# A two-layer kernel with a causal convolution in front: layer 1's 128-column down products in float32r parts, low parts made by transfers

## The chip, the cores and the metric
The kernel runs on one core of one Trainium2 chip. The time is that of the device in microseconds, from one launch to its end; three runs of the kernel before give a median of 1350.51 us (1350.42 to 1352.89). All operands and results are float32 in HBM.

## What is computed
The input is x (2, 4096, 192). A depthwise causal convolution with 7 taps comes first, its weights a softmax over the taps of each of 8 heads of 24 features. Two layers follow on the 8192 tokens, each 192 to 2048 to 192:

```python
x1 = conv(x, softmax(weight))
h = x1 @ w_in1;  g1 = h * (1 / (1 + exp(-1.702 * h)));  x2 = g1 @ w_out1
h = x2 @ w_in2
P = a0 + a1*h + a2*h**2 + a3*h**3
Q = 1 + abs(b0)*abs(h) + abs(b1)*h**2
out = (P / (Q + 1e-6)) @ w_out2
```

## The kernel before
Tokens are handled in 16 tiles of 512 (index i), and the 2048 hidden features in 16 blocks of 128, two at a time, a duo. A tile has eight steps (s = 0 to 7), one for each duo; n = 8 i + s numbers them. All tensors stand with features on the partitions and tokens along the row.

Step n does, on TensorE in this order (`step`, L365): the up products of layer 1 for duo n (`up`, L285: per block four full products of float32r, then `up_rest`, L294, a 64-row one), those of layer 2 for duo n - 10, and then the down products, of layer 2 for duo n - 12 and of layer 1 for duo n - 1. A down product has a 64-column part (`down_b`, L314, fp32; both layers side by side in one bank) and a 128-column part. For layer 2 the latter is fp32 (`down_a`, L299). For layer 1 it is `down_a` in two duos of eight and in all of tile 0, and `down_a_split` (L306) in the six duos of `S_SPLIT`: there the first block is one fp32 product (L309), and the second is made of three float32r products (L310 to L312), of the high and low parts of weights and g: hi x hi, lo x hi, hi x lo. An fp32 product stands in the trace as two records.

ScalarE reads h of layer 2 three times (`linear`, L510; Square, L525; Abs, L527), does layer 1's Gelu (L533), rounds the second block of g to float32r (`g_hi`, L536), and for the ratio P/Q makes two squares (L574, L576) and a seed of the reciprocal from Q's bits (L581). VectorE makes the numerator (L713, L715), Q (L716), two steps of the ratio (L735, L739, the latter writes g of layer 2), the last factor (L748), `g_lo` = g - g_hi (L764), and the taps of the next tile's convolution (`conv_ops`, L638, spread over the steps by the table `CONV_AT`). GpSimd makes m = Q x seed once a step (L858), which needs ScalarE's Abs and is needed by L574. SP's queue holds only loads and stores of tiles (`tile_io`, L257). Layer 2's input needs layer 1's sums: high parts by ScalarE (L540) and VectorE (L706), low parts by VectorE (L708, L742), at s = 0.

x is transposed on TensorE at s = 7 (half 0) and s = 0 (half 1), the result y at s = 5 and 6; ScalarE evacuates them in the same step, between its Gelu and L574, and splits x1 at s = 6. `y_a` and `y_b` are copied from the sums at s = 3. Tiles 0 to 2 and the last ones are written out; the ten tiles between run in a loop of two tiles (`Fori`) on every engine. The last ten duos of layer 2 run alone.

All orders are written out by hand through the numbers at the top (lags, `S_...`, `CONV_AT`) and semaphores; there is no scheduler.

## Time and profile before

| | before |
|---|---|
| median of 3 runs | 1350.51 us (1350.42 to 1352.89) |
| the profiled execution | 1351.36 us, its span 1348.9 us |
| instructions | 15463 |
| VectorE busy | 1180.0 us in 1323 instructions |
| ScalarE busy | 1023.6 us in 1235 instructions |
| GpSimd busy | 322.5 us in 147 instructions |
| bytes moved by DMA | 20.56 MB, mean 15 GB/s |

The span is the time from the first to the last instruction on the core; all times in rows count from its start. Busy time is the union of the instructions of an engine; matmuls overlap, so that distances between their starts say more than their lengths.

### The profile page before, as it was taken

Reading aid. Unit: us, or ns where it says so; the run is one execution under the profiler, and the core shown is the slowest. Engines: PE = TensorE matmul, PEld = TensorE weight load, DVE = VectorE, ACT = ScalarE, POOL = GpSimd, SP = SyncE. Lnnn points to the kernel's source line nnn. Section 1 sums busy time; section 2 is a strip of 40 time slices with the busy share of each in tenths; the row PEclk is TensorE's granted clock in tenths of the full one; section 3 lists DMA queues with packets and bytes.
Section 4 is the critical chain, followed back from the end, with each engine's and each line's share of the span. In section 5 each row is a group of like instructions: output and inputs, shape, how many; then the busy total and the mean of one; then the engine's idle time right before and its main releaser. Section 6 shows DMA issues by size and latency. Waiting matters only on the chain. (4 is left out here: it accounts for less than half of the span.)

```text
span 1348.9 us, 15463 instructions
## 1 busy us (share of the span) xinstructions
PE 1306.8 (97%) x4902; PEld 714.3 (53%) x4902; DVE 1180.0 (87%) x1323; ACT 1023.6 (76%) x1235; POOL 322.5 (24%) x147
## 2 busy tenths in 40 slices
PE   5998999999999999999999999999999999999896
PEld 3554555555555555555555555555555555555432
DVE  4469898989989898998989999898999989987897
ACT  4357778787877877787877878788787877877675
POOL 2312222222222222222222222222222222222231
PEclk9999999999999999999999999999999999999899
DMA  7200000000000000000000000000000000000000
GB/s 190 76 0 0 12 1 24 1 24 1 12 12 0 24 0 24 0 12 12 0 24 0 23 0 12 12 0 24 0 12 12 1 12 1 12 0 12 1 12 12
DMA packets 32922, 20.56 MB, mean 15 GB/s; under 512 B 10337, under 2 KB 30817, under 8 KB 32865
## 3 DMA queue, kind: packets, MB, share of 16 engines
q1 hardware_dynamic: 32388, 19.93, 5.3%
q8 instruction: 19, 0.31, 0.1%
q14 instruction: 38, 0.31, 0.1%
q10 hardware_dynamic: 477, 0.01, 0.0%
HBM read 13.64 MB, written 6.29 MB: 15 GB/s over the span
## 5 line engine op out<-in xcount | busy, mean ns | idle before, releaser
L858 POOL TENSOR_TENSOR work<-work 128x1024 f32<-128x1024 f32 x127 | 302.9, 2385 | 973.8 <-ACT work L527 927.1
L303 PE MATMUL acc_a<-g,down 128*128 128x512 f32 x664 | 312.3, 600 | 0.0
L317 PE MATMUL acc_b<-g,down 128*64 128x512 f32 x992 | 256.9, 608 | 17.4 <-DVE g L739 13.5
L514 ACT ACTIVATE work<-h,par 128x1024 f32<-128x1024 f32 x128 | 142.7, 1115 | 160.2 <-PE h L297 159.7
L289 PE MATMUL h<-x_a_hi,up_a_hi 128*128 128x512 f32 x512 | 234.3, 458 | 8.8 <-DVE x_a_lo L742 4.9
L713 DVE TENSOR_TENSOR work<-work,h 128x1024 f32<-128x1024 f32 x128 | 156.2, 1221 | 76.3 <-ACT work L527 75.1
L574 ACT ACTIVATE work<-work 128x1024 f32<-128x1024 f32 x127 | 134.9, 1062 | 96.3 <-POOL work L858 96.0
L290 PE MATMUL h<-x_a_lo,up_a_hi 128*128 128x512 f32 x512 | 201.0, 393 | 0.0
L291 PE MATMUL h<-x_a_hi,up_a_lo 128*128 128x512 f32 x512 | 200.9, 392 | 0.0
L292 PE MATMUL h<-x_b,up_b_hi 128*128 128x512 f32 x512 | 200.5, 392 | 0.0
L303 PEld LDWEIGHTS acc_a<-g,down 128*128 128x128 f32 x664 | 121.6, 189 | 142.8 <-issue 134.6
L715 DVE SCALAR_TENSOR_TENSOR work<-work,par,h 128x1024 f32<-128x1024 f32 x128 | 163.9, 1281 | 4.5
L739 DVE SCALAR_TENSOR_TENSOR g<-work 128x1024 f32<-128x1024 f32 x127 | 155.7, 1226 | 12.5 <-DVE work L735 1.9
L748 DVE SCALAR_TENSOR_TENSOR work<-work,par 128x1024 f32<-128x1024 f32 x128 | 163.7, 1279 | 1.1 <-ACT work L581 1.1
L735 DVE SCALAR_TENSOR_TENSOR work<-work 128x1024 f32<-128x1024 f32 x127 | 154.8, 1219 | 7.1 <-ACT work L574 7.0
L716 DVE SCALAR_TENSOR_TENSOR work<-work 128x1024 f32<-128x1024 f32 x128 | 156.1, 1220 | 0.0
L533 ACT ACTIVATE g<-h 128x1024 f32<-128x1024 f32 x128 | 132.5, 1035 | 30.2 <-PE h L297 30.2
L317 PEld LDWEIGHTS acc_b<-g,down 128*64 128x64 f32 x992 | 65.7, 136 | 143.4 <-issue 124.0
L581 ACT ACTIVATE work<-work 128x1024 int32<-128x1024 int32 x128 | 133.6, 1044 | 7.9 <-DVE work L716 7.9
L576 ACT ACTIVATE work<-work 128x1024 f32<-128x1024 f32 x127 | 132.6, 1044 | 0.0
L527 ACT ACTIVATE work<-h 128x1024 f32<-128x1024 f32 x128 | 131.1, 1024 | 0.0
L525 ACT ACTIVATE work<-h 128x1024 f32<-128x1024 f32 x128 | 129.9, 1015 | 0.0
(117 smaller groups left out, 1418.3 us busy)
## 6 DMA issues: line engine op xcount, KB each, us to landing
out<-y_out SPq DMA_DIRECT2D x15, 384.0 KB, 2.5
x_in_a<-in_x SPq DMA_DIRECT2D x16, 256.0 KB, 2.8
down<-in_moe_w_out SPq DMA_DIRECT2D x8, 384.0 KB, 6.3
...
work<-in_moe_w_in SPq DMA_DIRECT2D x8, 256.0 KB, 4.3
...
wts<-in_weight ACTq DMA_DIRECT2D x2, 0.4 KB
```

What stands on the lines that cost most here:

```text
L289: mm(h, l.up_a_hi[:, cols], l.x_a_hi[:, p, :], start=True, stop=False)
L290: mm(h, l.up_a_hi[:, cols], l.x_a_lo[:, p, :], start=False, stop=False)
L291: mm(h, l.up_a_lo[:, cols], l.x_a_hi[:, p, :], start=False, stop=False)
L292: mm(h, l.up_b_hi[:, cols], l.x_b[:, p, :], start=False, stop=False)
L303: last = mm(l.acc_a[:], l.down[:, f, 0:P], l.g[:, slot, k, :], start=f == 0, stop=f == STEPS - 1)
L317: return mm(acc_b[l.acc_row:l.acc_row + DB, :], l.down[:, f, P:D], l.g[:, slot, k, :], start=f == 0, stop=f == STEPS - 1)
L713: tt(tu, tu, h, ALU.mult).then_inc(t2_ready, 1)
L715: stt(tu, tu, par[:, 1:2], h, ALU.add, ALU.mult).then_inc(t3_ready, 1)
L716: stt(sk, ab, 1.0 + 1e-6, sk, ALU.add, ALU.add).then_inc(q_ready, 1)
L739: stt(gv, s2, d2, zv, ALU.add, ALU.mult).then_inc(g2_ready, 1)
L748: stt(zu, tu, par[:, 0:1], seed, ALU.add, ALU.mult).then_inc(z1_ready, 1)
L858: tt(m, sq[(s - LAG_RATIO) % 2], seed, ALU.mult).then_inc(m_ready, 1)
```

## The change
All 128-column down products of layer 1 are made of float32r parts, for both blocks of every duo and in tile 0 too: six products in place of four or two. The signs are turned: the weights have parts `down_nhi` = -hi, `down_nlo` and `down_hi`, and g has `g_nhi` = -hi. The low part of g is `g_low` = g + g_nhi. In tile 0 VectorE adds it; from tile 1 on two plain transfers on SP's queue copy g to `g_low`, and two adding transfers on GpSimd's queue add `g_nhi` onto it. Layer 2's fp32 products now stand ahead of layer 1's. z shares t1's buffers, and s2 those of sq, which frees room. Transpositions of x go to s = 5 and 6, of y to s = 0 and 1 of the tile after; ScalarE evacuates at the end of the step before. x1 is split at s = 4 and 5. The taps stand at s = 6 and 7 (of the tile after next) and s = 1, 2, 3. The loops are gone.

```diff
-S_XT = (7, 0)
-S_X1 = 6
+S_XT = (5, 6)
+S_X1_B = 4
+S_X1_A = 5
+S_X1_LO = 5
-S_SPLIT = (1, 2, 3, 4, 5, 7)
-S_YT = (5, 6)
+S_YT = (0, 1)
+S_LOAD = 3
-    CONV_AT = (0, 3, 8, 11, 14, 17, NX, NX, NX)
-    CONV_AT_FIRST = (0, 0, 0, 0, 7, 14, NX, NX, NX)
+    CONV_HEAD = {6: (0, 7), 7: (7, 10)}
+    CONV_AT = (10, 10, 13, 16, NX, NX, NX, NX, NX)
+    CONV_AT_FIRST = (0, 0, 0, 3, 10, NX, NX, NX, NX)
...
+            for n in range(END):
+                i, s = n // DUOS, n % DUOS
+                if live(n) and n >= DUOS:
+                    sp.wait_ge(g1_ready, n + 1)
+                    for k in range(2):
+                        sp.dma_start(g_low[:, n % 2, k, :].bitcast(F32), L1.g[:, n % 2, k, :]).then_inc(g1_copied[2 * (n % 2) + k], 16)
...
-            def down_a_split(d, slot):
-                acc = L1.acc_a[:]
-                mm(acc, L1.down[:, 2 * d, 0:P], L1.g[:, slot, 0, :], start=d == 0, stop=False)
-                mm(acc, down_hi[:, d, :], g_hi[:, slot, :], start=False, stop=False)
-                mm(acc, down_lo[:, d, :], g_hi[:, slot, :], start=False, stop=False)
-                return mm(acc, down_hi[:, d, :], g_lo[:, slot, :], start=False, stop=d == DUOS - 1)
+            def down_a_parts(v, slot):
+                acc = L1.acc_a[:]
+                for k in range(2):
+                    f = 2 * (v % DUOS) + k
+                    if v >= DUOS:
+                        pe.wait_ge(g1_low[2 * slot + k], 16 * ((v - DUOS) // 2 + 1))
+                    elif k == 0:
+                        pe.wait_ge(g1_low_first, v + 1)
+                    mm(acc, down_nhi[:, f, :], g_nhi[:, slot, k, :], start=f == 0, stop=False)
+                    mm(acc, down_nlo[:, f, :], g_nhi[:, slot, k, :], start=False, stop=False)
+                    done = mm(acc, down_hi[:, f, :], g_low[:, slot, k, :], start=False, stop=f == STEPS - 1)
+                return done
...
+            def linear(n, k):
+                act.wait_ge(h2_ready, k + 1)
+                if k - 2 + LAG_UP2 >= TOTAL - 1:
+                    wait(act, z1_ready, k - 1)
+                else:
+                    wait(act, g2_ready, k - 1)
...
+                    act.wait_ge(g1_ready, n + 1)
+                    fn(g_nhi[:, n % 2, :, :], L1.g[:, n % 2, :, :], ACT.Copy, scale=-1.0).then_inc(g1_nhi_ready, 1)
...
+                if n < DUOS:
+                    dve.wait_ge(g1_nhi_ready, n + 1)
+                    tt(g_low[:, n % 2, :, :], L1.g[:, n % 2, :, :], g_nhi[:, n % 2, :, :].bitcast(F32), ALU.add)\
+                        .then_inc(g1_low_first, 1)
+                    if s < CHUNKS:
+                        down_lo(s)
...
+                if live(n) and n >= DUOS:
+                    pool.wait_ge(g1_nhi_ready, n + 1)
+                    for k in range(2):
+                        pool.wait_ge(g1_copied[2 * (n % 2) + k], 16 * ((n - DUOS) // 2 + 1))
+                        pool.dma_start(g_low[:, n % 2, k, :], g_nhi[:, n % 2, k, :], accum_op=ALU.add)\
+                            .then_inc(g1_low[2 * (n % 2) + k], 16)
```

TensorE's down products of one middle step, with numbers for the layer or the bank behind a name (acc_a1 is layer 1's sum). Before, a split step:

```order
L317 MATMUL acc_b<-g2,down2 64x512 [waits g2_ready,g1_ready]
L317 MATMUL acc_b<-g1,down1 64x512
L317 MATMUL acc_b<-g2,down2 64x512
L317 MATMUL acc_b<-g1,down1 64x512
L309 MATMUL acc_a1<-g1,down1 128x512 [waits g1_lo_ready]
L310 MATMUL acc_a1<-g_hi,down_hi 128x512
L311 MATMUL acc_a1<-g_hi,down_lo 128x512
L312 MATMUL acc_a1<-g_lo,down_hi 128x512
L303 MATMUL acc_a2<-g2,down2 128x512 x2
```

Of the change, the same place:

```order
L350 MATMUL acc_b<-g2,down2 64x512 [waits g2_ready,g1_ready]
L350 MATMUL acc_b<-g1,down_b1 64x512
L350 MATMUL acc_b<-g2,down2 64x512
L350 MATMUL acc_b<-g1,down_b1 64x512
L330 MATMUL acc_a2<-g2,down2 128x512 x2
L343 MATMUL acc_a1<-g_nhi,down_nhi 128x512 [waits g1_low_0]
L344 MATMUL acc_a1<-g_nhi,down_nlo 128x512
L345 MATMUL acc_a1<-g_low,down_hi 128x512
L343 MATMUL acc_a1<-g_nhi,down_nhi 128x512 [waits g1_low_1]
L344 MATMUL acc_a1<-g_nhi,down_nlo 128x512
L345 MATMUL acc_a1<-g_low,down_hi 128x512
```

Layer 2's pair moved ahead of layer 1's products, which wait once for each half's transfer.

GpSimd's queue in the change, two middle steps (work<-work is m; before, only those rows stood here):

```order
L885 TENSOR_TENSOR work<-work 128x1024 [waits s2_ready,h2_read,seed_ready]
L891 DMA g_low<-g_nhi 128x512 [waits g1_copied_0,g1_nhi_ready]
L891 DMA g_low<-g_nhi 128x512 [waits g1_copied_1]
L885 TENSOR_TENSOR work<-work 128x1024 [waits s2_ready,h2_read,seed_ready]
L891 DMA g_low<-g_nhi 128x512 [waits g1_copied_2,g1_nhi_ready]
L891 DMA g_low<-g_nhi 128x512 [waits g1_copied_3]
```

Each m now stands behind the two adding transfers of the step before, and they behind SP's copies.

## Rows read from the trace of the kernel before
**Rows 1.** The page, busy time and share of the span of each engine.
```profile
PE 1306.8 (97%) x4902; PEld 714.3 (53%) x4902; DVE 1180.0 (87%) x1323; ACT 1023.6 (76%) x1235; POOL 322.5 (24%) x147
PEclk9999999999999999999999999999999999999899
```
**Rows 2.** Windows (stretch: length, busy PE, PEld, DVE, ACT, POOL, clock, DMA): middle tile, tile 2, tile 1.
```profile
617.06:696.51 79.45, 79.14 (x309) 44.12 (x308) 72.64 (x82) 63.28 (x76) 19.02 (x8) 1.00 0.03 10
140.61:219.94 79.33, 79.09 (x307) 44.17 (x307) 71.93 (x82) 63.23 (x76) 19.00 (x8) 1.00 0.04 11
64.57:140.61 76.04, 70.49 (x257) 38.38 (x257) 62.03 (x68) 48.16 (x55) 13.02 (x5) 1.00 0.03 9
```
**Rows 3.** Timeline of TensorE, two middle steps: start, length, line [idle before <- releaser].
```profile
640.98 1.88 PE L303 MATMUL acc_a<-g,down 128*128 128x512 f32 x4
642.92 0.39 PE L290 MATMUL h<-x_a_lo,up_a_hi 128*128 128x512 f32 x1
...
646.45 0.73 PE L297 MATMUL h<-x_b,up_b_lo 64*128 64x512 f32 x4
647.11 1.94 PE L317 MATMUL acc_b<-g,down 128*64 128x512 f32 x8
...
656.11 0.73 PE L297 MATMUL h<-x_b,up_b_lo 64*128 64x512 f32 x4
```
**Rows 4.** Timeline of ScalarE and VectorE in one step (s = 2 of a middle tile).
```profile
637.59 1.11 ACT L514 ACTIVATE work<-h,par 128x1024 f32<-128x1024 f32 x1 [1.69 <-PE h L297]
...
640.41 1.04 ACT L533 ACTIVATE g<-h 128x1024 f32<-128x1024 f32 x1
640.63 1.22 DVE L713 TENSOR_TENSOR work<-work,h 128x1024 f32<-128x1024 f32 x1 [0.59 <-ACT work L527]
641.47 0.63 ACT L536 ACTIVATE g_hi<-g 128x512 fp32r<-128x512 f32 x1
643.01 1.07 ACT L574 ACTIVATE work<-work 128x1024 f32<-128x1024 f32 x1 [0.90 <-POOL work L858]
645.53 1.23 DVE L739 SCALAR_TENSOR_TENSOR g<-work 128x1024 f32<-128x1024 f32 x1
646.67 1.28 DVE L748 SCALAR_TENSOR_TENSOR work<-work,par 128x1024 f32<-128x1024 f32 x1
```
**Rows 5.** Timeline at s = 0, the step after it, and s = 4.
```profile
617.95 1.12 ACT L514 ACTIVATE work<-h,par 128x1024 f32<-128x1024 f32 x1 [1.75 <-PE h L297]
621.25 1.22 DVE L713 TENSOR_TENSOR work<-work,h 128x1024 f32<-128x1024 f32 x1
627.62 1.94 PE L317 MATMUL acc_b<-g,down 128*64 128x512 f32 x8 [0.17 <-DVE g L739]
...
656.98 0.20 PEld L317 LDWEIGHTS acc_b<-g,down 128*64 128x64 f32 x4 [0.57 <-ACT y_a L593]
```
**Rows 6.** Groups by line (busy us, mean ns | idle before).
```profile
L764 DVE TENSOR_TENSOR g_lo<-g,g_hi 128x512 fp32r<-128x512 f32 x90 | 61.6, 684 | 2.2 <-ACT g_hi L536 2.2
L841 POOL TENSOR_TENSOR up_a_lo<-work,up_a_hi 128x512 fp32r<-128x512 f32 x7 | 9.4, 1336 | 32.3 <-DVE x_b L687 17.8 <-ACT up_b_hi L508 14.5
```
**Rows 7.** DMA issues (KB each, median us to landing), and the window of the fastest transfers.
```profile
x_in_a<-in_x SPq DMA_DIRECT2D x16, 256.0 KB, 2.8
down<-in_moe_w_out SPq DMA_DIRECT2D x8, 384.0 KB, 6.3
32.00:40.00 8.00, 8.00 (x29) 3.69 (x25) 0.96 (x5) 4.76 (x8) 2.56 (x2) 1.00 0.96 282
```
**Rows 8.** Timeline of VectorE in tile 1: taps, and the numerator's first operation of two steps.
```profile
98.47 0.74 DVE L656 SCALAR_TENSOR_TENSOR conv_a<-xt_a,wts,conv_a 128x512 f32<-128x512 f32 x1
99.13 0.47 DVE L656 SCALAR_TENSOR_TENSOR conv_b<-xt_b,wts,conv_b 128x256 f32<-128x256 f32 x1
99.53 2.86 DVE L656 SCALAR_TENSOR_TENSOR conv_a<-xt_a,wts,conv_a 128x512 f32<-128x512 f32 x1
...
102.31 1.21 DVE L713 TENSOR_TENSOR work<-work,h 128x1024 f32<-128x1024 f32 x1
...
113.72 1.21 DVE L713 TENSOR_TENSOR work<-work,h 128x1024 f32<-128x1024 f32 x1
```

More of the change, by code:

```diff
@@ L116, in build_program @@
             l.acc_a = pb("acc_a" + n, [P, NT])
-        down_hi = sb("down_hi", [P, DUOS, P], F32R)
-        down_lo = sb("down_lo", [P, DUOS, P], F32R)
-        g_hi = sb("g_hi", [P, 2, NT], F32R)
-        g_lo = sb("g_lo", [P, 2, NT], F32R)
+        L1.down_b = sb("down_b1", [P, STEPS, DB])
+        down_hi = sb("down_hi", [P, STEPS, P], F32R)
+        down_nhi = sb("down_nhi", [P, STEPS, P], F32R)
+        down_nlo = sb("down_nlo", [P, STEPS, P], F32R)
+        g_nhi = sb("g_nhi", [P, 2, 2, NT], F32R)
+        g_low = sb("g_low", [P, 2, 2, NT], F32R)
+        L2.down = sb("down2", [P, STEPS, D])
+        L2.down_b = L2.down[:, :, P:D]
         up_b_lo = sb("up_b_lo", [P, FF], F32R)
@@ L183, in live @@
         def live(duo):
-            return not isinstance(duo, int) or 0 <= duo < TOTAL
+            return 0 <= duo < TOTAL
         def alone(n):
-            return isinstance(n, int) and n >= TOTAL
+            return n >= TOTAL
         def last(duo):
-            return isinstance(duo, int) and duo == TOTAL - 1
+            return duo == TOTAL - 1
         def h2_banks(n):
@@ L461, in _ @@
                 mm(L1.acc_a[:], ident[:], xt_a[:, HALO:], start=True, stop=True)
-            for i in range(FIRST):
-                for s in range(DUOS):
-                    step(i, s, i % 2)
-            with pe.Fori(0, (LAST - FIRST) // 2) as j:
-                for o in range(2):
-                    for s in range(DUOS):
-                        step(j * 2 + (FIRST + o), s, (FIRST + o) % 2)
-            for i in range(LAST, TILES + 2):
+            for i in range(TILES + 2):
                 for s in range(DUOS):
@@ L608, in _ @@
             weights_hi(L1, 1, stage1, w1_hi)
-            split_x1(0, 0)
-            for i in range(FIRST):
+            x1_b_hi(0, 0)
+            x1_a_hi(0, 0)
+            for i in range(TILES + 2):
                 if i == 1:
@@ L618, in _ @@
                     step(i, s, i % 2)
+                    if i == 0 and s < CHUNKS:
+                        down_parts(s)
                     if i == 0 and s < 2:
                         weights_hi(L1, 2 + s, stage1, w1_hi)
-                    if i == 0 and s == DUOS - 2:
-                        fn(down_hi[:], L1.down[:, 1::2, 0:P], ACT.Copy).then_inc(down_hi_done, 1)
                     if i == 0 and s in S_WEIGHTS2:
                         weights_hi(L2, S_WEIGHTS2.index(s), stage2, w2_hi)
-            with act.Fori(0, (LAST - FIRST) // 2) as j:
-                for o in range(2):
-                    for s in range(DUOS):
-                        step(j * 2 + (FIRST + o), s, (FIRST + o) % 2)
-            for i in range(LAST, TILES + 2):
-                for s in range(DUOS):
-                    step(i, s, i % 2)
         @block.vector
@@ L652, in tap @@
                     if k == 0:
-                        wait(dve, x1_hi_done, 4 * tile)
-                        wait(dve, x1_lo_done, 3 * tile)
+                        wait(dve, (x1_a_hi_done, x1_b_hi_done)[part], (1, 3)[part] * tile)
+                        wait(dve, (x1_a_lo_done, x1_b_lo_done)[part], (1, 2)[part] * tile)
                         return ts(acc[:], src, w, None, ALU.mult)
@@ L761, in step @@
-                if s in S_SPLIT and live(n) and not (isinstance(i, int) and i == 0):
-                    slot = (s - LAG_GELU) % 2
-                    dve.wait_ge(g1_hi_ready, len(S_SPLIT) * (i - 1) + S_SPLIT.index(s) + 1)
-                    tt(g_lo[:, slot, :], L1.g[:, slot, 1, :], g_hi[:, slot, :].bitcast(F32), ALU.subtract)\
-                        .then_inc(g1_lo_ready, 1)
-                if s == S_X1 and tile_live(i + 1):
-                    split_x1(i + 1, 1 - p)
+                    if alone(n + 1):
+                        dve.wait_ge(g2_ready, u)
@@ L768, in step @@
+                if s == S_X1_LO and tile_live(i + 1):
+                    x1_lo(i + 1, 1 - p)
                 for op in conv[at[s]:at[s + 1]]:
                     op().then_inc(conv_steps, 1)
[L771 to L778 removed]
+                if s in CONV_HEAD and tile_live(i + 2):
+                    for op in conv_ops(i + 2)[slice(*CONV_HEAD[s])]:
+                        op().then_inc(conv_steps, 1)
@@ L823, in _ @@
             ts(root[:, 2:3], root[:, 1:2], 1.0, None, ALU.mult).then_inc(root_ready, 1)
-            for i in range(FIRST):
-                tile_steps(i, i % 2)
-            with dve.Fori(0, (LAST - FIRST) // 2) as j:
-                for o in range(2):
-                    tile_steps(j * 2 + (FIRST + o), (FIRST + o) % 2)
-            for i in range(LAST, TILES + 2):
-                tile_steps(i, i % 2)
+            for i in range(TILES + 2):
+                conv = conv_ops(i + 1) if tile_live(i + 1) else []
+                at = CONV_AT if i else CONV_AT_FIRST
+                for s in range(DUOS):
+                    step(i, s, i % 2, conv, at)
         @block.gpsimd
```

438 lines of the change are left out of this document (219 added, 219 removed).

## The prediction
> **What bounds the kernel now.** I read the page's busy shares first: TensorE is busy 97% of the span at full granted clock, VectorE 87%, ScalarE 76%, GpSimd 24% [rows 1]. Then the windows by tile, because the ends of the program have other limits: a middle tile takes 79.4 us, and TensorE is busy for 79.1 of them; tile 2, which stands outside the loop, takes 79.3 [rows 2]. Then TensorE's timeline: in a split step the rows follow each other with no idle note, and from one `up_rest` group (L297) to the next there are 9.66 us [rows 3]. So a middle step is as long as TensorE's stream, and a product is priced by the distance between starts, not by its recorded length, which overlaps the next one. Two fp32 down products of layer 2 start at 640.98; L290 starts at 642.92, and L289 ahead of it takes one place of 0.23, so the two took 642.92 - 0.23 - 640.98 = 1.71 us, 0.86 each. Float32r products stand 0.23 apart [rows 3].
>
> VectorE and ScalarE are close behind [rows 4]. I write H for the end of a step's up products (ScalarE's L514 starts there, 637.59). GpSimd's product and VectorE's L713 start at H+3.0, the Gelu (L533) ends at 641.45, H+3.9, and then ScalarE waits 0.90 us for GpSimd. VectorE's L748 ends 7.3 us after L713 began (647.95), 0.7 us into the next step, and the taps follow. Of TensorE's waits in a tile two count: 0.17 us for VectorE's g after s = 0, and about 0.2 at s = 4, where L317 starts 0.87 us behind L297 (656.98, 656.11) in place of 0.66 (647.11, 646.45), released by ScalarE's `y_a` [rows 3, 5]. What is left of 79.45 - 8 x 9.66 - 2 x 0.17 (the unsplit steps) - 0.37 are 1.46 us for twelve transpositions, 0.12 each.
>
> **TensorE's products.** A split step's layer-1 part is one fp32 and three float32r products, 0.86 + 3 x 0.23 = 1.55 us; an unsplit one 2 x 0.86 = 1.72. Six float32r products take 1.38. The saving is 0.17 in each of six steps and 0.34 in the other two, 1.70 us a tile. The 64-column products, the up products and the number of transpositions stay.
>
> **ScalarE.** The negated copy of all of g (128x1024) replaces one of 128x512 in six steps of eight. A pass over 128x1024 takes 1.04, as L533, the half of it 0.63. The 0.41 more falls between the Gelu and L574, where ScalarE waits 0.90 us for GpSimd [rows 4]. In the two unsplit steps evacuations and splits stood there, which move to the ends of steps, where 1.69 us are idle ahead of L514 [rows 4]. Cost: nothing; without that cover it would be 0.4 to 1.0 us a step. At s = 0 `x_a_hi` of layer 2 now waits for the layer-1 products at the end of TensorE's step: 640.98 - 1.55 - 637.59 + 1.71 + 1.38 = H+4.9, and ends near H+5.7, where L574 could start at H+5.4. VectorE is later than that at s = 0 anyway (below), so nothing is charged. `linear` (L552) now waits for g2 of the duo before last, since z lies in t1's buffer. That g2 (L739) is ready at 646.76, 0.5 us before the next L514 [rows 4]; the event is the one that TensorE's L317 waits for already.
>
> **VectorE.** It loses `g_lo`, 0.68 us in each of 90 steps [rows 6]. Steps s = 1, 2, 3 and 7 get three taps without it, at most 0.66 + 0.40 + 0.74 = 1.8 us (a, b, a; starts 98.47, 99.13, 99.53) [rows 8], so a step's work is 7.3 + 1.8 = 9.1 us against 9.5 of stream. The end of the taps comes at 0.7 + 0.17 (the shorter step) + 1.8 = H+2.7, GpSimd's product at H+3.0: 0.3 us to spare. At s = 7 three taps come ahead of layer 2's x parts, so L713 at s = 0 moves from H+3.3 (621.25 against 617.95) [rows 5] to about H+3.8, and g2 to H+10.0. TensorE's step there is 9.49 + 3 x 0.12 for transpositions that stand there now, 9.8. The old wait of 0.17 grows by 0.1 us a tile.
>
> **Other waits of the stream.** `y_a` at H+9.7 meets a step of 9.49, so the wait at s = 4 grows by 0.2 us. The loop goes: tile 2 needed 79.33, looped tiles 79.4 [rows 2], so -0.1 a tile.
>
> **The transfers.** From tile 1 on each step has two plain copies of 256 KB on SP's queue, issued at the Gelu's end, and two adding ones on GpSimd's, each behind its copy. No row shows an adding transfer, or one issued by GpSimd. The first half is needed by the layer-1 products of the next step, now behind layer 2's: 640.98 - 1.55 + 9.66 + 1.71 - 0.17 = 650.6, 9.1 us after the Gelu's end; the second is due 0.69 later, at 9.8 [rows 3, 4]. A 256 KB load lands in 2.8 us, and at 282 GB/s, the fastest stretch, one behind it lands 0.9 later [rows 7]. GpSimd's issue is bounded by nothing and by 1.34, its 128x512 operation [rows 6]; I take 1.3, the bad end. The adding transfer is bounded below by nothing (an earlier landing changes no sum) and above by 6.3 (384 KB in the crowded start) [rows 7]; I take the 2.8 of the load of its own size, plus 0.9 for the one in front. First half: 2.8 + 1.3 + 2.8 = 6.9, so 2.2 to spare. Second half: 2.8 + 1.3 + 1.3 + 2.8 + 0.9 = 9.1, so 0.7 to spare. Cost: nothing. On SP's queue a waiting copy holds back only tile loads and stores, which have steps of time. On GpSimd's queue the wait for the copies ends near H+7.6 and the issues by H+9.5, 3 us before its next product.
>
> The Trainium skill ("DMA: Bandwidth & Descriptors", Anatomy of one DMA) fits a GpSimd-issued transfer as 2.0 us plus its bytes at 436 GB/s. That is an estimate of 2.6 us for 256 KB; no run here shows it. By it the second half would have 0.9 us to spare, the sum would be the same, and the late case below would get 0.12 instead of 0.17.
>
> **The ends.** Tile 0 had fp32 products only: 8 x 0.34 = 2.7 us saved. Against that VectorE gets eight additions and four subtractions (8 x 1.2 + 4 x 0.68 = 12.3 us, by the lengths of L713 and L764) and eleven taps in one step, and TensorE waits for the first low weights: taken -1, from -3 to +4. Tile 1 took 76.0 us [rows 2], although only six of its steps have layer 2: some four steps took about 11.4 (L713 at 102.31 and 113.72), because the last tap met GpSimd's product and ran 2.86 us in place of 0.74 [rows 8]. Without `g_lo` that should not start: 4 x (11.4 - 9.66) = 7 gone, less a first wait for transfers in the two short steps; taken -5, from -9 to +3. The last ten duos of layer 2 are VectorE's and stay.
>
> **Sum.** Tiles 2 to 15: 14 x (-1.70 + 0.1 + 0.2 - 0.1) = -21.0. Tile 1: -5. Tile 0: -1. Together -27, from a profiled time of 1351.4: 1324.4. The median of the runs is 0.9 lower, so **1323.5 us**. With the good ends (no wait grows, tile 1 -9, tile 0 -3) it is 1350.5 - 14 x 1.9 - 12 = 1312; with the bad ones (half of 21, tile 1 +3, tile 0 +4) 1347.
>
> **Rivals.** *Late low parts (slower).* If the adding transfer takes the 6.3 us of the crowded row, the second half lands at 2.8 + 2.6 + 6.3 = 11.7, 1.9 us late. TensorE stands ahead of the layer-1 products with the next up products queued behind them. From the Gelu of a duo to the up products of the duo after next lie two steps, so a step grows by half the lateness: 0.95 x 120 = 114, less the 27, makes 1437 us. Gain turns to loss at 0.45 us of lateness. For it: no row prices the transfer. Against: 0.7 to 2.2 us to spare.
> *GpSimd's issues hold VectorE (slower).* A tap was held for 2.1 us by GpSimd [rows 8]. If an issue of 1.3 us holds VectorE once a step, its work is 9.1 + 1.3 = 10.4 against 9.66: 0.74 x 120 = 89, 1439 us. Against: the issues fall at H+7.6 to H+9.5, not on GpSimd's long read.
> The Trainium skill ("SBUF — State Buffer", Who interferes with whom) says that a VectorE instruction with two SBUF inputs contends with a GpSimd one that reads SBUF; the trace agrees, 2.86 against 0.74 [rows 8]. It infers that issuing a transfer needs only the write side, which no run here shows; by that this rival would be nothing.
> *The gain is given back in part.* With margins of 0.3 us VectorE and ScalarE set the steps with taps, and half of the 21 us comes: 1335.
> *No change.* One tap of a tile is held after all, because 0.3 us to spare are not there: 14 x (2.1 - 0.3) = 25, so 1349.
>
> **Chances.** Forecast 0.57, given back in part 0.12, no change 0.05, late low parts 0.17, VectorE held 0.09. A measurement can tell about 0.2% here, 2.7 us. Faster 0.69, same 0.05, slower 0.26. The range goes from 1310 to 1390: 0.03 lies below, and 0.17 above, the greater part of both slow cases. The likeliest case alone is 1310 to 1347.
>
> **What would show it.** Right: L297's successors 9.5 us apart, tiles of 77 to 78.5 us, no idle note ahead of the first `down_nhi` product, adding transfers landed within 9 us of the Gelu's end, taps at 0.74 throughout, tile 1 near 71. Wrong: TensorE waiting for `g_low` in each step; VectorE's rows stretched by 1 to 2 us beside GpSimd's product or issues; ScalarE's L552 waiting for g2 in most steps.

## The result and the profile after

The change takes 1338.68 us (median of 4 runs, 1337.28 to 1341.83) against 1350.97 for the kernel before on the same chip (4 runs): ratio 0.9912, 95% interval 0.99 to 0.9923. That is faster by 12 us; 27 were forecast. The lines below are from the page of the change: the busy shares, the clock, two groups (busy us, mean ns | idle before) and the two kinds of transfer (KB each, median us from the start of the issue to landing). They are the counterpart of [rows 1, 6, 7]:

```profile
PE 1280.2 (96%) x5068; PEld 748.1 (56%) x5068; DVE 1131.5 (85%) x1244; ACT 1105.3 (83%) x1280; POOL 535.3 (40%) x387
PEclk9999999999999999999999999999999999999898
L891 POOL DMA_DIRECT2D g_low<-g_nhi x240 | 211.5, 1012 | 190.3 <-DMA g_low<-g 183.8
L343 PE MATMUL acc_a<-g_nhi,down_nhi 128*128 128x512 f32 x256 | 149.1, 582 | 2.1 <-DMA g_low<-g_nhi 2.1
g_low<-g SPq DMA_DIRECT2D x240, 256.0 KB, 2.4
g_low<-g_nhi POOLq DMA_DIRECT2D x240, 256.0 KB, 3.7
```

TensorE was busy 26.6 us less, near what the sum has, but its share fell from 97 to 96%: half of the gain came back as idle time. GpSimd waited 183.8 us for the copies, which held nobody; TensorE waited 2.1 us in all for transfers, three times, all in tile 1.

I cut both spans at the same places: the start of each step's `up_rest` rows (L297 before, L324 in the change). The windows of the change (columns as in [rows 2]) are tile 0, tile 1, a middle tile, and everything behind the start of the last layer-1 step:

```profile
21.66:69.09 47.43, 41.93 (x164) 24.91 (x163) 29.34 (x48) 30.30 (x44) 15.97 (x13) 0.96 0.33 94
69.09:142.29 73.20, 69.65 (x267) 41.33 (x266) 50.85 (x61) 52.55 (x57) 26.20 (x21) 0.98 0.48 115
532.80:610.85 78.05, 77.34 (x317) 46.06 (x316) 68.97 (x76) 67.91 (x78) 32.59 (x24) 1.00 0.49 116
1232.11:1336.90 104.79, 81.05 (x220) 35.57 (x219) 82.60 (x75) 66.64 (x81) 24.39 (x11) 0.93 0.06 17
```

The same windows of the kernel before, for tile 0 and the end:

```profile
21.38:64.57 43.19, 42.08 (x149) 21.58 (x148) 16.57 (x28) 18.48 (x28) 16.94 (x13) 1.00 0.37 102
1249.51:1348.90 99.39, 80.84 (x216) 34.92 (x215) 82.87 (x76) 65.27 (x77) 23.70 (x10) 0.93 0.02 8
```

| stretch, us | before | change | difference | forecast |
|---|---|---|---|---|
| start, to the first `up_rest` | 21.38 | 21.66 | +0.3 | 0 |
| tile 0 | 43.19 | 47.43 | +4.2 | -1 |
| tile 1 | 76.04 | 73.20 | -2.8 | -5 |
| tiles 2 to 15 | 1108.90 | 1089.82 | -19.1 | -21 |
| from the last layer-1 step on | 99.39 | 104.79 | +5.4 | 0 |
| span | 1348.9 | 1336.9 | -12.0 | -27 |

So the middle is near the forecast and the ends are not: 12.8 of the 15 us missing lie in tile 0, tile 1 and the end. Four places of the change's timeline say why.

**Tile 0**, VectorE, GpSimd, ScalarE and TensorE around its step 4:

```profile
43.32 1.36 POOL L872 TENSOR_TENSOR up_b_lo<-work,up_b_hi 64x512 fp32r<-64x512 f32 x1
43.45 1.38 DVE L684 TENSOR_SCALAR conv_b<-xt_b,wts 128x256 f32<-128x256 f32 x1
44.89 0.75 DVE L685 SCALAR_TENSOR_TENSOR conv_a<-xt_a,wts,conv_a 128x512 f32<-128x512 f32 x1
...
52.50 0.16 DVE L688 TENSOR_SCALAR xt_b<-halo_b 64x6 f32<-64x6 f32 x1
52.70 0.60 ACT L517 ACTIVATE xt_a<-turned 128x512 f32<-128x512 f32 x1 [7.90 <-DVE xt_b L688]
54.23 1.01 ACT L569 ACTIVATE g<-h 128x1024 f32<-128x1024 f32 x1
55.39 0.47 PE L316 MATMUL h<-x_a_hi,up_a_hi 128*128 128x512 f32 x1 [1.60 <-ACT g L569]
```

VectorE works through its taps from 44.89 to 52.50, with one addition of 1.22 us between them. ScalarE's evacuation of tile 2's input (L517) overwrites what the taps read, so it waits 7.90 us for the last of them, and the next Gelu stands behind it in ScalarE's order. TensorE then waits for that Gelu. Before, the evacuation came three steps later.

**Tile 1**, the first duo with transfers, its two halves:

```profile
73.82 1.90 POOL L891 DMA_DIRECT2D g_low<-g_nhi  x2 [11.50 <-DMA g_low<-g]
77.43 0.47 PE L343 MATMUL acc_a<-g_nhi,down_nhi 128*128 128x512 f32 x1 [0.67 <-DMA g_low<-g_nhi]
79.49 0.50 PE L343 MATMUL acc_a<-g_nhi,down_nhi 128*128 128x512 f32 x1 [1.13 <-DMA g_low<-g_nhi]
80.21 0.63 PE L345 MATMUL acc_a<-g_low,down_hi 128*128 128x512 f32 x1
```

The two steps without layer 2 take 5.1 us each, shorter than a copy, an issue and an adding transfer together. Behind the waits the records are 0.63 long in place of 0.40: the granted clock of 80 to 90 us is 0.84, part of the time at 1.2 GHz.

How much of this step is the clock can be read from the run e_tail, whose program is the same up to the end of layer 1. The step with the two waits, in the change and in e_tail:

```profile
74.18:85.63 11.45, 9.65 (x30) 5.86 (x30) 1.46 (x4) 2.08 (x2) 3.24 (x4) 0.85 0.67 139
75.70:85.55 9.85, 8.05 (x31) 4.74 (x30) 1.46 (x4) 2.08 (x2) 3.26 (x4) 1.00 0.66 141
```

At full clock the step takes 9.85 us. So of the change's 11.45 the lower clock is 1.6, and the waits are the 2.1 over the 7.73 us that the step takes without transfers (e_no_transfers, below). In e_tail the low clock fell earlier, in tile 0 (0.85 over 43 to 62 us), and tile 0 took 49.0 us. Tiles 0 and 1 together are 120.6 us in both, so these two tiles trade 1.6 us with each other from run to run.

**A middle tile** has the two waits that the prediction had, at s = 1 and s = 4:

```profile
543.62 0.61 PE L350 MATMUL acc_b<-g,down 128*64 128x512 f32 x1 [0.26 <-DVE g L774]
572.54 0.61 PE L350 MATMUL acc_b<-g,down 128*64 128x512 f32 x1 [0.45 <-ACT y_a L607]
```

Its steps are 9.83, 9.80, 9.45, 9.48, 10.47, 9.73, 9.45 and 9.84 us, in all 78.05.

**The end**, where layer 2 runs alone. First the change, then the kernel before, at the same place:

```profile
1304.18 1.23 DVE L774 SCALAR_TENSOR_TENSOR g<-work,x_in 128x1024 f32<-128x1024 f32 x1
1305.44 1.02 ACT L563 ACTIVATE work<-h 128x1024 f32<-128x1024 f32 x1 [0.33 <-DVE g L774]
1306.36 1.02 ACT L565 ACTIVATE work<-h 128x1024 f32<-128x1024 f32 x1
1307.48 1.22 DVE L746 TENSOR_TENSOR work<-work,h 128x1024 f32<-128x1024 f32 x1 [0.65 <-ACT work L565]
```

```profile
1317.48 1.23 DVE L739 SCALAR_TENSOR_TENSOR g<-work 128x1024 f32<-128x1024 f32 x1
1317.93 1.00 ACT L525 ACTIVATE work<-h 128x1024 f32<-128x1024 f32 x1
1318.84 1.01 ACT L527 ACTIVATE work<-h 128x1024 f32<-128x1024 f32 x1
1319.95 1.22 DVE L713 TENSOR_TENSOR work<-work,h 128x1024 f32<-128x1024 f32 x1
```

In the change s2 lies in sq, so the Square (L563) may overwrite it only when g (L774) has read it. The Abs comes after it, and VectorE idles 0.65 us for the Abs. Before, the Square ran beside g. Steps here take 8.20 us for 7.5.

### The profile page after: what moved, and what is told of

Same layout as the page of the kernel before. It is cut to its first block and busy times, and to the rows that moved or that the text cites. A ratio compares the mean times of both kernels' runs of the same rounds, so it can differ in the third digit from the quotient of the medians.

```text
span 1336.9 us, 15156 instructions
## 1 busy us (share of the span) xinstructions
PE 1280.2 (96%) x5068; PEld 748.1 (56%) x5068; DVE 1131.5 (85%) x1244; ACT 1105.3 (83%) x1280; POOL 535.3 (40%) x387
## 5 line engine op out<-in xcount | busy, mean ns | idle before, releaser
L891 POOL DMA_DIRECT2D g_low<-g_nhi x240 | 211.5, 1012 | 190.3 <-DMA g_low<-g 183.8
L330 PE MATMUL acc_a<-g,down 128*128 128x512 f32 x512 | 254.7, 620 | 0.0
L350 PE MATMUL acc_b<-g,down_b 128*64 128x512 f32 x480 | 231.6, 605 | 0.0
L552 ACT ACTIVATE work<-h,par 128x1024 f32<-128x1024 f32 x128 | 142.6, 1114 | 96.7 <-PE h L324 81.6
L316 PE MATMUL h<-x_a_hi,up_a_hi 128*128 128x512 f32 x512 | 208.1, 407 | 13.4 <-DVE x_a_lo L777 5.5
L588 ACT ACTIVATE work<-work 128x1024 f32<-128x1024 f32 x127 | 134.8, 1061 | 71.8 <-POOL work L885 71.8
L330 PEld LDWEIGHTS acc_a<-g,down 128*128 128x128 f32 x512 | 87.1, 190 | 166.3 <-issue 166.3
L774 DVE SCALAR_TENSOR_TENSOR g<-work 128x1024 f32<-128x1024 f32 x117 | 143.4, 1226 | 10.6
L343 PE MATMUL acc_a<-g_nhi,down_nhi 128*128 128x512 f32 x256 | 149.1, 582 | 2.1 <-DMA g_low<-g_nhi 2.1
L784 DVE SCALAR_TENSOR_TENSOR work<-work,par 128x1024 f32<-128x1024 f32 x117 | 149.6, 1279 | 1.1 <-ACT work L594 1.1
L571 ACT ACTIVATE g_nhi<-g 128x1024 fp32r<-128x1024 f32 x128 | 136.0, 1063 | 4.0
```

The lines of the kernel that those rows point to most:

```text
L316: mm(h, l.up_a_hi[:, cols], l.x_a_hi[:, p, :], start=True, stop=False)
L330: done = mm(L2.acc_a[:], L2.down[:, f, 0:P], L2.g[:, slot, k, :], start=f == 0, stop=f == STEPS - 1)
L350: return mm(acc_b[l.acc_row:l.acc_row + DB, :], l.down_b[:, f, :], l.g[:, slot, k, :], start=f == 0, stop=f == STEPS - 1)
L784: stt(z_of(u), tu, par[:, 0:1], seed, ALU.add, ALU.mult).then_inc(z1_ready, 1)
L891: pool.dma_start(g_low[:, n % 2, k, :], g_nhi[:, n % 2, k, :], accum_op=ALU.add)\
```

## The experiments

All are edits of the change. The table has their stretches, cut as above, of the profiled run, and the median of the timed runs with its ratio to the kernel before (95% interval).

| run | tile 0 | tile 1 | tiles 2 to 15 | the end | span | median | ratio |
|---|---|---|---|---|---|---|---|
| change | 47.4 | 73.2 | 1089.8 | 104.8 | 1336.9 | 1338.7 | 0.9912 (0.99 to 0.9923) |
| e_tail | 49.0 | 71.6 | 1089.9 | 100.8 | 1333.0 | 1334.8 | 0.9879 (0.9862 to 0.9897) |
| e_tile0 | 44.9 | 71.6 | 1089.7 | 105.2 | 1334.5 | 1335.7 | 0.989 (0.9873 to 0.9908) |
| e_tile0_spread | 42.8 | 73.2 | 1090.0 | 106.4 | 1334.1 | 1333.4 | 0.9865 (0.9849 to 0.9882) |
| e_first10 | 47.4 | 69.5 | 1089.9 | 106.5 | 1335.1 | 1338.1 | 0.9906 (0.9889 to 0.9922) |
| e_no_transfers | 47.7 | 69.5 | 1089.4 | 105.1 | 1334.6 | 1335.7 | 0.989 (0.9872 to 0.9908) |
| e_vector_low | 46.0 | 74.0 | 1229.9 | 106.4 | 1477.8 | 1479.9 | 1.095 (1.0929 to 1.097) |
| e_half_fp32 | 47.9 | 71.8 | 1100.9 | 106.3 | 1348.6 | 1349.9 | 0.9991 (0.9982 to 1.0001) |
| e_order | 47.5 | 73.3 | 1103.9 | 103.7 | 1350.1 | 1351.9 | 1.0006 (0.9997 to 1.0015) |
| e_ya | 47.5 | 73.2 | 1084.7 | 105.2 | 1332.3 | 1335.1 | 0.9882 (0.9865 to 0.9898) |
| e_head9 | 49.0 | 71.7 | 1085.7 | 106.8 | 1334.8 | 1334.8 | 0.9879 (0.9864 to 0.9894) |
| e_best | 42.8 | 69.5 | 1085.2 | 100.5 | 1319.6 | 1321.4 | 0.9788 (0.9773 to 0.9803) |
| e_best_taps | 42.8 | 69.5 | 1080.6 | 100.9 | 1315.5 | 1317.3 | 0.9748 (0.9734 to 0.9761) |

Stretches that an edit does not touch show the noise of one profile: the end goes from 104.8 to 106.8 and tile 0 from 46.0 to 49.0, while tiles 2 to 15 repeat within 0.7 us. Where tile 0 took 49.0 us, tile 1 took 1.6 less than in the change, by the clock as above. The start is 21.6 to 21.7, but 22.9 and 23.0 in e_no_transfers and e_tile0. So the ends are judged by their own stretch and its rows, the middle by its tiles.

### The end: e_tail
```diff
-        z_alone = x_in
+        z_alone = (L1.g[:, 0, :, :], x_in[:])
+        def s2_of(k):
+            return L1.g[:, 1, :, :] if k + LAG_RATIO > TOTAL else sq[k % 2]
...
-                    wait(act, g2_ready, k - 1)
+                    if k - 2 + LAG_RATIO > TOTAL:
+                        wait(act, m_ready, k - 1)
+                    else:
+                        wait(act, g2_ready, k - 1)
                     fn(sq[k % 2], h2_banks(n)[:], ACT.Square, scale=scale_root)
...
                     if alone(n + 1):
-                        dve.wait_ge(g2_ready, u)
+                        dve.wait_ge(g2_ready, u - 1)
...
```


> The change, but in the steps behind the last layer-1 duo z has two buffers and layer 2's s2 a buffer of its own again (both in memory of layer 1 that is free by then), and the waits that the shared ones brought are gone. Theory A (the shared buffers make each of the last steps 8.2 us in place of 7.45, because ScalarE's Square waits for VectorE's g and VectorE then for ScalarE's Abs): the stretch behind step 128 shrinks from 104.8 to about 99.4 us, 1338.7 becomes 1333.3 (1332 to 1335), and no idle note stands ahead of VectorE's L746 row there. Theory B (the end is longer because GpSimd and ScalarE got slower there or the first step behind the last layer-1 duo changed, not through the buffers): 1338 to 1339, steps of 8.2 us stay.

The end shrank by 4.0 us, from 104.8 to 100.8, and the median by 3.9. The rows at the same place, Square, Abs and VectorE's first operation:

```profile
1301.94 1.02 ACT L570 ACTIVATE work<-h 128x1024 f32<-128x1024 f32 x1
1302.85 1.03 ACT L572 ACTIVATE work<-h 128x1024 f32<-128x1024 f32 x1
1303.98 1.22 DVE L758 TENSOR_TENSOR work<-work,h 128x1024 f32<-128x1024 f32 x1 [0.49 <-ACT work L572]
```

Steps are 7.3 to 7.6 us again. The Square no longer waits for g; here y's evacuation stands ahead of it, so a wait of 0.49 stays. Theory A holds for 4.0 of its 5.4; the run gives both buffers back at once, so it does not split z from s2, and only the rows name the Square and s2. Of the other 1.4, 0.8 is one step: the last layer-1 step takes 15.4 us for 14.6, because `x_a_hi` of the last tile waits for layer 1's products, which now stand behind layer 2's (e_best turns them round for this duo and has 14.6).

### Tile 0: e_tile0 and e_tile0_spread
```diff
+            if i == 0 and s in (6, 7):
+                return (2, s - 6)
-            if s in S_XT and i >= 0 and tile_live(i + 2):
+            if s in S_XT and i > 0 and tile_live(i + 2):
...
+                head = CONV_HEAD if i else {7: (0, 10)}
...
```


> The change, but in tile 0 the transpositions and evacuations of tile 2's input stand in steps 6 and 7 in place of 5 and 6, and the ten operations on it at VectorE all in step 7. Theory A (in tile 0 the evacuation on ScalarE waits for the last of eleven taps, 7.9 us, and holds the Gelu of the next step): tile 0 shrinks from 47.4 us to 43 to 44, total 1334.5 to 1335.5. Theory B (tile 0 is held by VectorE's own work, additions and taps, in whatever order): tile 0 stays above 46.5 and the time at 1338 to 1339. Either way a wait for the later load or the later transpositions may come back in tile 1, at most 1 us.

Tile 0 took 44.9 us (2.5 less), above theory A's 43 to 44, and its step of 9.6 us became one of 8.8 a step later: ScalarE again waited for the last tap, now 4.88 us:

```profile
56.29 0.60 ACT L519 ACTIVATE xt_a<-turned 128x512 f32<-128x512 f32 x1 [4.88 <-DVE xt_b L690]
```

Tile 1 took 71.6 us, 1.6 less than in the change, its second step at full clock (9.84 us). So the wait moved and shrank; the rest needed the taps themselves spread.

```diff
-    CONV_AT_FIRST = (0, 0, 0, 3, 10, NX, NX, NX, NX)
+    CONV_AT_FIRST = (0, 0, 0, 3, 8, 14, NX, NX, NX)
+    CONV_AT_SECOND = (0, 10, 13, 16, NX, NX, NX, NX, NX)
...
+            if n in (DUOS - 1, DUOS):
+                return (2, n - DUOS + 1)
...
```


> The change, but in tile 0 the taps of tile 1's input are spread 5, 6 and 7 over steps 3, 4 and 5 in place of 7 and 11 over two, x1's split stands one step later, and the transpositions of tile 2's input move to the last step of tile 0 and the first of tile 1. The run with transpositions in steps 6 and 7 took 44.9 us for tile 0, with one step of 8.8 us, where the evacuation again waited for the last tap. Theory A (that wait on ScalarE is what holds the Gelu): tile 0 becomes 42 to 43 us, total 1333 to 1334.5. Theory B (VectorE's additions and taps fill tile 0 in any order): tile 0 stays at 44 to 45 or tile 1 grows by what tile 0 loses, total 1335 to 1336.5.

Tile 0 took 42.8 us, 4.6 less than the change and 0.4 less than the kernel before; tile 1 kept its 73.2. The window of tile 0 in this run:

```profile
21.67:64.50 42.83, 39.84 (x163) 24.17 (x162) 30.14 (x39) 30.42 (x44) 17.14 (x13) 1.00 0.37 104
```

The first operations on tile 2's input, four taps among them, moved on to tile 1, but VectorE is busy for 30.1 us of tile 0, against 29.3 in the change. Theory A: it was the order, not VectorE's load. A wait of 3.04 us for the last tap stays and makes one step 7.1 us. The clock, 0.96 in the change's tile 0, is 1.00 here, so a part of the 4.6 is the lower clock that came with the wait. The median is 5.3 lower.

### The transfers: e_no_transfers, e_first10, e_order, e_vector_low
e_no_transfers removes both transfers of each half and the waits for them.

```diff
-                    if v >= DUOS:
-                        pe.wait_ge(g1_low[2 * slot + k], 16 * ((v - DUOS) // 2 + 1))
-                    elif k == 0:
+                    if v >= DUOS and k == 0:
+                        pe.wait_ge(g1_nhi_ready, v + 1)
+                    elif k == 0:
...
```


> The change without its transfers of the low parts of g (neither copies nor adding ones; from tile 1 on the products read an old low part, so this part of the computation is left out; every product is still made). Theory A (the transfers are hidden but for the first duos of tile 1, where TensorE waits 2.1 us for them): 1336 to 1337.5, middle tiles 77.9 to 78.0 us, tile 1 some 1 to 2.5 us shorter. Theory B (the 480 transfers and their issues on GpSimd cost the middle tiles, through stretched operations or late products): over 5 us less in all, middle tiles under 77.6 us.

A middle tile of that run:

```profile
530.50:608.54 78.04, 77.34 (x318) 46.06 (x317) 68.97 (x76) 67.91 (x78) 19.27 (x8) 1.00 0.04 11
```

78.04 against 78.05 us, with DMA at 11 GB/s in place of 116 and GpSimd 13 us less busy: in the middle the 480 transfers cost nothing that shows (0.5 us in fourteen tiles). Only the second step of tile 1 changed, 7.73 us for 11.45. That is theory A, though tile 1 gave 3.7 us where 1 to 2.5 were expected, and the median, 1335.7, lies just below its range.

e_first10 lets VectorE add in those two steps, and starts the transfers at the third (`DUOS` becomes 10 in four conditions and two counts; two conditions are shown).

```diff
-                if live(n) and n >= DUOS:
+                if live(n) and n >= 10:
...
-                if n < DUOS:
+                if n < 10:
                     dve.wait_ge(g1_nhi_ready, n + 1)
...
```


> The change, but VectorE makes the low parts of g also in the first two steps of tile 1, which have no layer 2 beside them and are 5 us short, and the transfers begin at the third. Theory A (a transfer pair takes longer than a short step, and the wait for it is the only cost of the transfers): the second step of tile 1, 11.46 us in the change, becomes 8 to 8.6; tile 1 becomes 69.5 to 70.5, total 1335 to 1336.5. Theory B (TensorE waits there for something else that is late, such as the first layer-2 weights or the x parts): 1338 to 1339.

Tile 1 became 69.5 us, as without transfers, and its second step 7.73: theory A there. Of these 3.7 us, 1.6 are the lower clock. But the median fell by 0.6 only, to where theory B had it. The end of this run's profile took 1.7 us more than the change's; windows (the change first, then e_first10), then VectorE's last g and TensorE's last products:

```profile
1312.00:1327.00 15.00, 11.52 (x20) 3.84 (x21) 13.63 (x15) 8.40 (x12) 2.35 (x1) 0.77 0.08 26
...
1325.87 1.29 DVE L766 SCALAR_TENSOR_TENSOR g<-work,x_in 128x512 f32<-128x512 f32 x2
...
1328.21 1.93 PE L350 MATMUL acc_b<-g,down 128*64 128x512 f32 x4
```

```profile
1308.00:1323.00 15.00, 10.05 (x15) 2.96 (x16) 13.63 (x14) 8.98 (x13) 2.35 (x1) 0.77 0.08 26
...
1322.46 1.29 DVE L766 SCALAR_TENSOR_TENSOR g<-work,x_in 128x512 f32<-128x512 f32 x2
...
1326.34 1.93 PE L350 MATMUL acc_b<-g,down 128*64 128x512 f32 x4
```

VectorE is in step in both. In the change the products start 1.05 us after g is there (1325.87 + 1.29), in e_first10 2.59 us after. TensorE was still busy with older products, slowed by the lower clock that both runs have after TensorE's idle stretch at the end, at slightly different moments. That takes 1.5 us back in this profile. Whether it does so in each run is open.

e_order puts layer 1's 128-column products ahead of layer 2's, 1.7 us earlier:

```diff
-                if live(v2):
-                    down_a(e2, slot2).then_inc(g2_used, 1)
                 if live(v1):
...
                     down_a_parts(v1, slot1).then_inc(g1_used, 1)
+                if live(v2):
+                    down_a(e2, slot2).then_inc(g2_used, 1)
```


> The change, but in each step the 128-column layer-1 products (float32r, with the low parts from the transfers) stand ahead of the two fp32 ones of layer 2 in place of behind them, so the low parts are due 1.71 us earlier: 9.1 - 1.7 = 7.4 and 8.1 us after the Gelu's end. Theory A (a plain copy of 256 KB lands in 2.4 us, an issue on GpSimd takes 0.88, an adding transfer lands in 3.7, as the change's profile has them: halves at 2.4 + 0.9 + 3.7 = 7.0 and 7.9 us): 0.2 to 0.4 us to spare on the median, a wait only for the longer ones; middle tiles 78.0 to 79.5, total 1337 to 1358, and the last step of layer 1 some 1 to 2 us shorter. Theory B (the step of transfers has little room even in the change's order): waits of 1 us or more in most steps, over 82 us a tile, over 1390 in all.

TensorE's waits for transfers, in the list of waits (us in total, times, longest):

```profile
PE acc_a L343 <- DMA g_low<-g_nhi: 12.9, 21, 1.4
```

Three of the 21 waits, 2.1 us, are those of tile 1, as in the change; the other 18, 10.8 us, lie in the 112 steps of tiles 2 to 15. It is theory A in kind, near the upper end of its time, with three tiles clearly past its 79.5 (79.9, 80.6 and 81.8).

How far the halves are from being late can be read from the landing times in the traces, tiles 3 to 15, counted from the end of the Gelu's row:

| | first half, median (latest) | second half, median (latest) | least time to the product |
|---|---|---|---|
| change | 6.2 (8.3) | 7.7 (9.8) | 0.94 and 0.35 us |
| e_order | 6.2 (8.6) | 7.7 (10.1) | 0.04 and 0.04 us, after waits |

So e_order's plain steps, which want the halves 7.4 and 8.2 us after the Gelu, have 1.2 and 0.5 us to spare at the median, and only the slower transfers are late, by 1.4 us at most. In the change's order even the slowest second half was 0.35 us early. What makes single transfers 1 to 2 us slower is not shown. The plain steps are also 9.51 us for 9.45; why is open. The whole gain of the change is gone in this order.

e_vector_low has no transfers; VectorE adds in all steps.

```diff
-                if n < DUOS:
+                if live(n):
                     dve.wait_ge(g1_nhi_ready, n + 1)
...
```


> The change with VectorE making the low parts of g (128x1024 additions of 1.17 us) in all steps, as it does in tile 0, and no transfers. Theory A (the transfers are what lets all products be float32r, since VectorE has only 0.3 us to spare in the steps with three taps): VectorE becomes the bound in steps with taps, its work of a middle tile is 0.85 x 78 + 8 x 1.17 = 75.7 but uneven, three taps steps 9.1 + 1.17 = 10.3 against 9.46, so four to five steps a tile grow by about 0.8 and some taps meet GpSimd's product and stretch: 81.5 to 86 us a tile, 1390 to 1450 in all. Theory B (VectorE's slack of 15% takes the additions): 78 to 79 us a tile, 1337 to 1350.

Window of a middle tile, and the third tap of s = 7 with GpSimd's product beside it:

```profile
853.08:941.93 88.85, 78.78 (x317) 46.10 (x316) 86.22 (x84) 68.46 (x79) 19.90 (x8) 1.00 0.03 9
...
857.75 2.45 POOL L879 TENSOR_TENSOR work<-work 128x1024 f32<-128x1024 f32 x1 [9.57 <-ACT work L559]
857.88 2.88 DVE L679 SCALAR_TENSOR_TENSOR conv_a<-xt_a,wts,conv_a 128x512 f32<-128x512 f32 x1
```

88.85 us a tile, past theory A's range, and 1480 us in all: the step in which that tap falls takes 13.8 to 15.5 us. The additions come to 8 x 1.22 = 9.8 us a tile, the loss is 10.8, and a tap that slides under GpSimd's product adds 2.1. The mechanism was right, the price too low: I counted only the steps with taps as late, but VectorE is 97% busy in this window (86.22 of 88.85), so it sets the whole tile.

### TensorE's products: e_half_fp32
```diff
+                    if k == 0:
+                        mm(acc, down_nhi[:, f, :].bitcast(F32), g_nhi[:, slot, k, :].bitcast(F32), start=f == 0, stop=False)
+                        continue
                     mm(acc, down_nhi[:, f, :], g_nhi[:, slot, k, :], start=f == 0, stop=False)
```


> The change, but the first half of each duo's 128-column layer-1 product is one fp32 product of the high parts in place of three float32r ones (its low parts are left out of the computation; transfers, copies and waits stay). By the distances between starts this puts 0.86 for 0.69 us, 0.17 a step. Theory A (TensorE's stream sets the middle steps and only two waits a tile, 0.34 at s = 1 and 0.45 at s = 4, take a longer step up): six of eight steps grow by 0.17, middle tiles 78.0 becomes 79.0 to 79.4, total 1354 to 1358. Theory B (the other engines set the steps, so the products' saving was given back there): middle tiles under 78.5, total under 1348.

```profile
456.98:535.75 78.77, 78.48 (x309) 44.50 (x308) 68.95 (x76) 67.85 (x78) 31.70 (x23) 1.00 0.48 115
```

Plain steps became 9.62 us for 9.45, the 0.17 that the distances between starts gave. The tile became 0.8 us longer, not 8 x 0.17 = 1.36, and not theory A's 1.0 to 1.4: at s = 1 the step fell from 9.80 to 9.62 (its wait for g is gone) and at s = 4 it stayed (10.46). So a product's price is right, and 0.5 us a tile of it is paid as waits once TensorE is that fast. The median, 1349.9, lies between the two theories.

### The two waits of the middle: e_ya and e_head9
```diff
-                        wait(pe, acc2_read, 3 * (v2 // DUOS))
+                        wait(pe, acc2_read, 3 * (v2 // DUOS) - 1)
...
                 if live(v2):
+                    if e2 == 0:
+                        wait(pe, acc2_read, 3 * (v2 // DUOS))
                     down_a(e2, slot2).then_inc(g2_used, 1)
```


> The change, but at the first duo of a tile's layer-2 down products TensorE waits for the two y_b copies alone ahead of the 64-column products, and for y_a only ahead of the 128-column ones. Theory A (the wait of 0.45 us at s = 4 is for y_a, and nothing stands behind it): middle step 10.46 becomes 10.0 to 10.1, middle tile 77.6, total 1332 to 1334. Theory B (the step is set there by ScalarE's chain or the next g too, so the wait moves on): total 1337 to 1339, a new wait for g or for x of the same size.

The step at s = 4 fell from 10.47 to 9.92, the one at s = 6 rose from 9.45 to 9.6, the tile became 77.65. Tiles 2 to 15 took 5.1 us less; the median fell by 3.6, to 1335.1, one us above theory A's range. Theory A, with a small part moved on.

```diff
-    CONV_HEAD = {6: (0, 7), 7: (7, 10)}
-    CONV_AT = (10, 10, 13, 16, NX, NX, NX, NX, NX)
+    CONV_HEAD = {6: (0, 7), 7: (7, 9)}
+    CONV_AT = (9, 9, 13, 16, NX, NX, NX, NX, NX)
```


> The change, but step 7 has two taps in place of three and step 1 four in place of three. Theory A (g2 is late for TensorE at s = 1 by 0.34 us because of the third tap in step 7, and a step takes three taps, 1.8 us, with 0.3 us to spare before GpSimd's product): step 1 gets 9.45 in place of 9.79, but the fourth tap of step 1 meets GpSimd's product, stretches from 0.74 to over 2 us and makes step 2 or 3 longer by 1 to 2 us: middle tiles 78.7 to 80, total 1348 to 1366. Theory B (VectorE has room for a fourth tap): middle tiles 77.65, total 1333 to 1335.

The first and last of the four taps of s = 1, and GpSimd's product behind them:

```profile
551.87 0.74 DVE L685 SCALAR_TENSOR_TENSOR conv_a<-xt_a,wts,conv_a 128x512 f32<-128x512 f32 x1
...
553.59 0.48 DVE L685 SCALAR_TENSOR_TENSOR conv_b<-xt_b,wts,conv_b 128x256 f32<-128x256 f32 x1
554.12 2.41 POOL L885 TENSOR_TENSOR work<-work 128x1024 f32<-128x1024 f32 x1 [4.09 <-ACT work L565]
```

My theory A fell on its second half: the last tap ends at 554.07, 0.05 us ahead of GpSimd's product, and nothing stretches. Step 1 became 9.46 us for 9.80 and no other grew; tiles are 77.7. The median is 1334.8, at theory B.

### All together: e_best and e_best_taps
e_best has e_tail, e_tile0_spread, e_ya and e_first10, and for the last duo of layer 1:

```diff
+                if last(v1):
+                    parts()
                 if live(v2):
...
-                if live(v1):
+                if live(v1) and not last(v1):
+                    parts()
```


> The change with all that the runs so far showed to help: two z buffers and an s2 of its own at the end, tile 0's taps spread over three steps, y_a waited for only by the 128-column products, VectorE's low parts in the first two steps of tile 1, and for the very last duo of layer 1 the layer-1 products ahead of layer 2's. Theory A (these act at different places and add up): 1338.7 - 3.9 (end) - 4.6 (tile 0) - 5.2 (y_a) - 3.7 (first transfers) - 1.0 (last duo) = 1320.3 us, 1318 to 1324 with the clock's ups and downs at the ends. Theory B (a gain at one end is given back by the clock or by the next wait): 1326 to 1333.

1321.4 us against 1320.3 expected (1318 to 1324): the edits add up. In the profile tile 0, tile 1, tiles 2 to 15 and the end are 4.6, 3.7, 4.6 and 4.3 us shorter than in the change, so e_first10's 3.7 is there too. e_best_taps adds the two lines of e_head9.

> The five edits of the last run together with the tap that moves from step 7 to step 1 (alone, that tap made a middle tile 77.7 us for 78.0). Theory A (the waits at s = 1 and s = 4 are apart, the edits add up): middle tiles 77.3, total 1321.4 - 14 x 0.33 = 1316.8 us, 1315 to 1320. Theory B (after y_a's wait is gone, the steps after s = 4 take a new wait for g, 9.6 in place of 9.45, and the moved tap makes that worse): middle tiles 77.6, 1320 to 1323.

```profile
520.93:598.27 77.34, 77.25 (x319) 45.98 (x318) 68.97 (x76) 67.92 (x78) 31.94 (x23) 1.00 0.49 117
```

1317.29 us (1315.31 to 1318.89, 5 runs), ratio 0.9748 (0.9734 to 0.9761), theory A: 2.5% faster than the kernel before, where the change is 0.9%. TensorE is idle 0.09 us in this tile.

## Where the prediction went wrong, and what held

It said faster, 1323.5 us, by 27. The direction held, the size did not: 12. The step that failed is the one on the ends of the program. "The last ten duos of layer 2 are VectorE's and stay" put the end at nothing, and it came at +5.4 us; tile 0, taken at -1, came at +4.2. Both are new waits in ScalarE's stream, made by a shared buffer and by a moved evacuation, which the prediction did not follow. Tile 1 adds 2.2 us that were missed. The price of the products, the waits of a middle tile and the hidden transfers held.

- **TensorE's products** (-1.70 a tile): the mechanism is right. Plain steps are 9.45 us for 9.49 forecast, and e_half_fp32 gives 0.17 for a step's half.
- **The waits of the middle** (+0.1 and +0.2): the places were right, the sizes 0.34 at s = 1 (0.27 forecast, with the old part) and 0.45 at s = 4 (0.4). A middle tile is 78.0, forecast 77.9, and tiles 2 to 15 gave 19.1 of 21.0. e_ya and e_head9 took each wait away.
- **The transfers** (nothing): right, and e_no_transfers shows it. The halves landed 6.2 and 7.7 us after the Gelu's end at the median of tiles 3 to 15, forecast 6.9 and 9.1. The parts were 2.4 us for a copy (2.8 taken), 0.88 for an issue (1.3), and 3.7 from the start of an adding transfer's issue to its landing. This last holds the issue, which the prediction added to it. What it had no term for is the spread: the slowest second half landed after 9.8 us and was 0.35 us early, so the margin was thinner than the 0.7 of the sum suggests. The rivals "late low parts" and "GpSimd's issues hold VectorE" did not come; e_order shows that with the products 1.7 us earlier the slow transfers take back the gain.
- **Tile 1** (-5, came -2.8): the taps stretched by GpSimd are gone, and the four steps of 11.0 to 11.6 us are 9.5 to 10.8, 5.8 us less in all where 7 were forecast. The term "less a first wait for transfers in the two short steps" had 2 us, and the step grew by 3.3, from 8.1 to 11.45. The transfers' own part, 2.1 us over the step without them, was sized right; the lower clock behind the waits, 1.6 us, had no term.
- **Tile 0** (-1, came +4.2, past the range's +4). The prediction named the eleven taps in one step but looked at VectorE's load alone. It did not follow the evacuation that moved ahead of them in ScalarE's order, nor who stands behind it. This is the part that failed first in time; e_tile0_spread shows 4.6 us of it.
- **The end** ("the last ten duos of layer 2 are VectorE's and stay", came +5.4). This sentence was wrong. It took VectorE's six operations as the bound, though the change put z and s2 into shared buffers, and I asked what the sharing does to L552 only in the middle. Alone, there is no TensorE work to hide the Square's wait for g. e_tail shows 4.0 of the 5.4, the turned order in e_best 0.8; 0.6 stays unexplained, within the end's noise.

The rival "given back in part" had 1335 us, near the time, but by margins in the middle steps. That is not what happened: those lost 2 us of 21. So the rival's time was near by luck. A slip without effect: the good end of the range has 14 x 1.9, where the terms give 14 x 1.8, 1313 us.

The Trainium skill ("DMA: Bandwidth & Descriptors", Anatomy of one DMA) gives by its fit 2.6 us for 256 KB issued by GpSimd, an estimate. The profile's median for the adding transfers is 3.7, so the measurement decides; it is 1.1 us more per adding transfer, and the sum would not change.

GpSimd's two issues beside VectorE operations with two SBUF inputs, in the change:

```profile
1231.06 1.22 DVE L770 SCALAR_TENSOR_TENSOR work<-work 128x1024 f32<-128x1024 f32 x1
1231.12 1.76 POOL L891 DMA_DIRECT2D g_low<-g_nhi  x2 [1.21 <-DMA g_low<-g]
1232.37 1.23 DVE L774 SCALAR_TENSOR_TENSOR g<-work 128x1024 f32<-128x1024 f32 x1
```

The first VectorE row began 0.06 us ahead of the issues and the second 0.51 us before their end. Both have their usual 1.22 and 1.23 us, while a tap of 0.74 us took 2.88 beside GpSimd's product. The Trainium skill ("SBUF — State Buffer", Who interferes with whom) infers that an issue needs only the write side and so does not hold such an instruction; the trace agrees.
